# Transposing the new q and k in halves of 64 rows, q's upper rows beside k's lower rows

## What is computed

```python
q_rot, k_rot = (rotate(q), rotate(k))
scores = scale * np.matmul(q_rot, k_rot.transpose(0, 1, 3, 2))
scores = scores - np.max(scores, axis=-1, keepdims=True)
attn = np.exp(scores)
attn = attn / (np.sum(attn, axis=-1, keepdims=True) + 1e-09)
x = np.matmul(attn, v)                       # then heads side by side: 2304 x 512
h = x @ w_in                                 # 512 x 2048
g = np.maximum(h, 0.0) + alpha * np.minimum(h, 0.0)
out = g @ w_out
```

## Time and profile before

| | us |
|---|---|
| median of 2 runs | 701.41 (700.92 and 701.91) |
| the profiled execution | 700.88 |
| its span | 699.1 |
| TensorE products busy | 676.6 (97%) |
| VectorE busy | 372.4 (53%) |
| ScalarE busy | 314.2 (45%) |
| GpSimd busy | 282.1 (40%) |
| moved by the transfers | 51.30 MB |

### The profile page before, as it was taken

The page is one execution under the profiler, slowest core; times in us unless marked ns, Lnnn a source line. Parts: engine busy times, 40 slices in busy tenths (PEclk is TensorE's granted clock), DMA queues, the critical chain, the costliest instruction groups (busy, mean ns, idle before and its releaser), DMA issues.

```text
span 699.1 us, 12111 instructions
## 1 busy us (share of the span) xinstructions
PE 676.6 (97%) x4100; PEld 588.0 (84%) x4100; DVE 372.4 (53%) x681; ACT 314.2 (45%) x740; POOL 282.1 (40%) x258
## 2 busy tenths in 40 slices
PE   3899999999999999899999999999999999999996
PEld 3788888888888887698889999999999999999995
DVE  4688888888888878445642333233233323432231
ACT  2777777777777776333332222322322232223222
POOL 6655777777776504122222222222222222222221
PEclk9999999999999999999999999999999999999999
DMA  6897656666666642600001000000000010001001
GB/s 154 220 225 195 147 135 140 142 146 143 143 143 145 148 106 79 239 1 0 1 1 46 0 1 16 31 0 1 30 15 0 0 43 2 0 0 46 2 0 46
DMA packets 76619, 51.30 MB, mean 73 GB/s; under 512 B 61088, under 2 KB 61472, under 8 KB 76064
## 3 DMA queue, kind: packets, MB, share of 16 engines
q1 hardware_dynamic: 76576, 50.76, 28.9%
HBM read 22.95 MB, written 4.72 MB: 40 GB/s over the span
## 4 chain that ended last, share of the span: by engine, by line
PE 76%; issue 16%; POOL 2%; DVE 2%; DMA 1%; ACT 1%; SPq 1%; POOLq 0%; DVEq 0%; ACTq 0%
PE banks L620 19%; PE banks L647 19%; PE banks L547 14%; PE banks L505 12%; PE banks L566 10%; POOL g_lo L449 2%; PE banks L562 2%; DVE nmax L846 1%; DMA k_two<-k_hi 0%; DMA cos_sb<-in_cos 0%; DMA out<-stage 0%; DVE pt L895 0%; DVE k_lo L871 0%; ACT stage L807 0%; SPq L294 0%
## 5 line engine op out<-in xcount | busy, mean ns | idle before, releaser
L449 POOL TENSOR_TENSOR g_lo<-g,g_hi 128x384 fp32r<-128x384 f32 x96 | 99.3, 1035 | 312.2 <-ACT g_hi L795 306.1
L960 DVE TENSOR_SCALAR g<-banks,alpha_sb 128x384 f32<-128x384 f32 x96 | 59.3, 618 | 249.1 <-ACT pos L787 249.1
L620 PE MATMUL banks<-x_hi,w_in_lo 128*128 128x384 f32 x384 | 129.3, 337 | 0.0
L620 PE MATMUL banks<-x_hi,w_in_hi 128*128 128x384 f32 x384 | 129.2, 336 | 0.0
L620 PE MATMUL banks<-x_lo,w_in_hi 128*128 128x384 f32 x384 | 129.0, 336 | 0.0
L787 ACT ACTIVATE pos<-banks 128x384 f32<-128x384 f32 x96 | 47.1, 491 | 169.1 <-PE banks L620 169.1
L846 DVE TENSOR_REDUCE nmax<-banks 128x1 f32<-128x576 f32 x144 | 108.6, 755 | 22.8 <-PE banks L505 17.6
L647 PE MATMUL banks<-w_out_hi,g_hi 128*128 128x512 f32 x288 | 114.9, 399 | 1.6 <-POOL g_lo L449 1.4
L647 PE MATMUL banks<-w_out_hi,g_lo 128*128 128x512 f32 x288 | 112.9, 392 | 0.0
L647 PE MATMUL banks<-w_out_lo,g_hi 128*128 128x512 f32 x288 | 111.9, 389 | 0.0
L795 ACT ACTIVATE g_hi<-g 128x384 fp32r<-128x384 f32 x96 | 50.5, 526 | 119.7 <-DVE g L963 119.7
(11 more groups left out here) (83 smaller groups left out, 909.8 us busy)
## 6 DMA issues: line engine op xcount, KB each, us to landing
k_two<-k_hi SPq DMA_DIRECT2D x64, 160.0 KB, 2.9
out<-stage SPq DMA_DIRECT2D x18, 256.0 KB, 2.0
raw_q<-in_q SPq DMA_DIRECT2D x32, 128.0 KB, 2.8
raw_k<-in_k SPq DMA_DIRECT2D x32, 128.0 KB, 2.4
q_two<-q_hi SPq DMA_DIRECT2D x32, 128.0 KB, 2.3
q_two<-q_lo SPq DMA_DIRECT2D x32, 128.0 KB, 2.3
q_own<-q_hi SPq DMA_DIRECT2D x32, 128.0 KB, 2.4
raw_v<-in_v SPq DMA_DIRECT2D x32, 128.0 KB, 2.3
```

The lines of the kernel that those rows point to most:

```text
L449: nc.gpsimd.tensor_tensor(g_lo[f % 2][:, :], g[f % 2][:, :], g_hi[f % 2][:, :].bitcast(F32), ALU.subtract).then_inc(g_lo_done, 1)
L620: mm = nc.tensor.matmul(h_ps[f % 2], w[:, j, cols], xx[:, j, :], start=(step == 0), stop=(step == 3 * CT - 1))
L960: nc.vector.tensor_scalar(g[f % 2][:, :], h_ps[f % 2], 0.0, alpha_sb[:, f:f + 1], ALU.min, ALU.mult).then_inc(neg_done, 1)
```

## The change

The eight transposes of U_Q and U_K (four blocks each, 128 rows by 128 columns) become sixteen of 64 rows by 128 columns. The moving operand is then a 64x64 corner of the identity, and one instruction fills 64 of the block's columns in the bank. They are made by a new function, `turn_new`, in two steps of eight: step 0 takes rows 0 to 63 of q and rows 64 to 127 of k in turns, step 1 takes the other two halves. Q's halves go to U_Q's bank (1) and k's to U_K's bank (2), so that neighbouring instructions use different rows of the array and different banks.

In a period, step 0 stands between A1 and U_PB[3], and step 1 between U_PB[3] and A2; U_MIXED stands directly behind A2, where U_K's transposes were before it. Ahead of A1 come the waits of both units: that both banks are free and that both `rot_q` and `rot_k` are ready. Between the two steps, ahead of U_PB[3], TensorE waits on a new semaphore, half_turned, that the last product of step 0 raises. The semaphore `turned` is raised by 2 at the end of step 1. At the start, for pair 0, the two steps follow each other, and both rotations are waited for first.

```diff
--- before.py
+++ after.py
@@ -217,7 +217,7 @@
         scored = sem("scored")
         max_done = sem("max_done")
         exp_done = sem("exp_done")
-        turned = sem("turned")
+        turned, half_turned = sem("turned"), sem("half_turned")
         hi_done = sem("hi_done")
         evac = [sem(f"evac{i}") for i in range(T_BANKS)]
         sum_done = sem("sum_done")
@@ -528,12 +528,6 @@
                 elif u == U_INV:
                     pe.wait_ge(wide_done, p)
                     blocks = [inv_wide[:, i, :] for i in range(QT)]
-                elif u == U_Q:
-                    turned_in(p, 0)
-                    blocks = [rot_q[:, i, :] for i in range(QT)]
-                elif u == U_K:
-                    turned_in(p, 1)
-                    blocks = [rot_k[:, i, :] for i in range(QT)]
                 else:
                     blocks = []
                     if has_next(p):
@@ -546,6 +540,24 @@
                     i = 2 if at else i
                     mm = nc.tensor.transpose(bank[:, i * P:(i + 1) * P], block_in, ident[:, :])
                 mm.then_inc(turned, 1)
+
+            def turn_new(p, t, step):
+
+                if not exists_now(p, U_Q):
+                    return
+                bank_q, bank_k = t_ps[U_Q % T_BANKS], t_ps[U_K % T_BANKS]
+                if isinstance(p, int) and p == -1:
+                    if step:
+                        pe.wait_ge(half_turned, 1)
+                    else:
+                        turned_in(p, 0)
+                        turned_in(p, 1)
+                low, high = slice(0, D), slice(D, P)
+                for i in range(QT):
+                    for bank, rot, rows in ((bank_q, rot_q, high if step else low), (bank_k, rot_k, low if step else high)):
+                        mm = nc.tensor.transpose(bank[:, i * P + rows.start:i * P + rows.stop], rot[rows, i, :],
+                                                 ident[rows, rows])
+                mm.then_inc(turned if step else half_turned, 2 if step else 1)
 
             def pv(p, par, h):
 
@@ -581,11 +593,18 @@
                 turn(p, t, U_PB[0])
                 turn(p, t, U_PB[1])
                 turn(p, t, U_PB[2])
+                if exists_now(p, U_Q):
+                    fill(p, U_Q)
+                    fill(p, U_K)
+                    turned_in(p, 0)
+                    turned_in(p, 1)
                 score(p, t, A_TILES[1])
+                turn_new(p, t, 0)
+                if exists_now(p, U_Q):
+                    pe.wait_ge(half_turned, p + 2)
                 turn(p, t, U_PB[3])
-                turn(p, t, U_Q)
+                turn_new(p, t, 1)
                 score(p, t, A_TILES[2])
-                turn(p, t, U_K)
                 turn(p, t, U_MIXED)
                 score(p, t, A_TILES[3])
                 if not has_now(p):
@@ -661,8 +680,9 @@
                     output(i, c, FT - 1)
 
             pe.wait_ge(ident_in, 16)
-            for u in (*OF_NEXT, U_MIXED):
-                turn(-1, -1, u)
+            turn_new(-1, -1, 0)
+            turn_new(-1, -1, 1)
+            turn(-1, -1, U_MIXED)
             pe.wait_ge(padded, PADDED)
 
             def batch(b):
```

## The result

The changed kernel takes 740.8 us as the median of two runs (739.56 and 742.04) against 701.41: a ratio of 1.0565 (95% interval 1.0531 to 1.0598). Timed again among the experiments it took 740.32 us over five runs, 733.19 to 743.36, a ratio of 1.0575 (1.0547 to 1.0603). That spread of 10 us, where the kernel before has 2, is part of the result: it comes from TensorE's clock.

The account below looks back on a forecast made before the run. TensorE, busy 97% of the span, was taken to bound the kernel. Fourteen periods at 2.02 us (28.3) plus 4.5 for the start, 32.8 on the profiled 700.88, gave 734 us; range 726 to 746.

Parts of the forecast that it names:

- the clock: Rival: idle 1.5 us each period drops TensorE's clock to 1.2 GHz, 1.5 us more per period, 755 us; chance 0.03.
- a period over 19 us: Sign that would make the prediction wrong; it expected a period of 18.6 us instead of 16.62.
- The bound: Middle periods: only TensorE's pieces on the chain of waits, so anything added to its queue lengthens the kernel one for one.
- The moved wait: A1's first product waits for ScalarE's copy of U_PB[2] out of bank 2; TensorE stands still 1.51 us a period.
- the 0.03 for the release: Time from the end of ScalarE's copy of U_PB[2] to A1's new start: 0.03 us.
- Changes of division and halves: Per period: four changes, half_turned wait included, 0.78 us; sixteen halves 0.60 (0.44 to 0.87); eight whole transposes saved, 0.87.
- the fear of the issue of 32 short instructions: Halves put at 0.6 us, not 0.44: 32 short loads and products must issue in the time of fewer than eight before.
- A middle period: Each of periods 1 to 14 grows by 2.02 us (1.72 to 2.29); fourteen give 28.3 us.
- The start: Start and period 0: A1 waits for rotated k, and shifts behind it add up to 4.5 us, ends 3 and 7.
- 1 us net: At the start, behind A1: halves with their changes and wait add some 1 us at TensorE's lower clock.
- the 0.9 of slack in the transfers: At the start, SyncE reached q's copies late, so 0.9 us of TensorE's delay would be taken up.
- the rival that followed from it: Halves cost as much as whole transposes because weight loads set the pace: 16 us more, 750 us; chance 0.09.

Follow-up runs that it names:

- e12: The changed kernel itself timed again, no edit: 740.32 us over five runs, 733.19 to 743.36; its execution without a clock fall spans 731.4 us.
- e1: The kernel before with only the waits for banks 1 and 2 and both rotations moved ahead of A1, transposes whole and in place: 726.72 us.
- e9: Against e3: halves in one stretch behind A2, lower rows to bank 1, upper to bank 2, no wait between; start as in the kernel before: 704.71 us.
- e3: The changed kernel with both steps behind A2, a whole transpose between them, and the bank and rotation waits on A2's last product: 713.68 us.
- e5: The changed kernel with the wait for half_turned carried by the last of U_PB[3]'s four transposes instead of the first: 733.83 us.
- e6: e3 with rows 0 to 63 of both q and k in step 0 and rows 64 to 127 of both in step 1: 723.15 us.
- e11: e3 with whole transposes in the old places at the start and in period 0, halves from period 1 on: 710.74 us.
- e10: The changed kernel with A1's four products made two extra times ahead of the moved waits, filling the idle stretch: 735.15 us.
- e7: e1 with three tiny activations ahead of ScalarE's copy of U_PB[2], lengthening TensorE's idle stretch: 734.62 us, runs from 730.64 to 739.38.
- e4: The changed kernel with four halves of q queued ahead of four of k in each step, instead of in turns: 742.40 us.
- e2: The changed kernel with its moved waits carried by the last of A1's four products instead of the first: 729.95 us.

## Why the prediction held, and where it didn't

The forecast was 734 us with a range of 726 to 746; the result is 740.8. That it lies inside is in part luck: the bounds added up from the terms ended at 740, the widening to 746 was for dearer halves, and what brought the result there is the clock, which had 3 in 100. One of the prediction's own signs of being wrong came true: a period over 19 us, in six periods of the profiled execution.

*The bound.* TensorE was alone on the chain, and what was added to its queue came out one for one. From period 14's U_INV to the end the kernel before takes 442.4 us (256.75 to 699.1) and e12 442.4 (289.02 to 731.4), so nothing was added behind the last period that the change touches.

*The moved wait,* 1.51 us forecast: e1 measures 1.79 in a middle and 1.55 in an end period, as what it adds to the period. The mechanism and ScalarE's run of five are as described (the copy ends 3.01 us after the run's start, in both traces). The mis-sized term is the 0.03 for the release: in the loop A1 starts 0.31 us after the end of the copy. In the unlooped code it is 0.11, by e12's timeline and chain: the copy is done at 244.18 + 0.61 = 244.79, and A1's piece begins at 244.90:

```profile
244.18 0.61 ACT L764 ACTIVATE pt<-banks 128x512 f32<-128x512 f32 x1
```

```profile
244.90 0.77 PE banks L505 x4
```

I had taken what a wait on a single thing shows; A1 now waits on four semaphores, in the loop against values in registers. That this is what takes the time is likely and not tested.

*Changes of division and halves,* 0.78 + 0.60 - 0.87 = 0.51 forecast: 18.82 - 18.41 = 0.41 against e1, and 18.58 - 18.17 = 0.41 in end periods. No run prices one change alone, but the terms fit: e9 and e3 differ by two changes and the wait, 0.44, where the forecast had 0.30 + 0.16. The halves took 8 x 0.06 = 0.48, nearer to the bound of 0.44 than to my 0.6; the fear of the issue of 32 short instructions was wrong. The wait for half_turned is smaller than its share (e5: 0.1 of the 0.30).

*A middle period,* 2.02 forecast: 2.16 as the mean of 13 in e12 ((289.02 - 44.92 - 256.75 + 40.69) / 13).

*The start,* 4.5 forecast: 2.7 at the first stacked tile of period 1 (2.5 in e12, at 34.80). A1 of period 0 came at 20.44 where 20.5 was said. The mis-sized term is the "1 us net" for the halves and their changes behind A1: they cost nothing up to A2 and save 0.8 up to A3, because k's first halves run beside A1's products and k's whole transposes are gone. No run shows that the 0.9 of slack in the transfers was used: A3 is 2.76 late and the first tile of period 1 2.67. The clock's part in it I can't separate.

*The sum,* 32.8 forecast, 32.3 in the execution without a fall: 2.5 for the start and 29.8 for the fourteen periods, where 4.5 and 28.3 were forecast. The start too long by 2 us and the periods too short by 1.5 nearly cancel, which is luck.

*The clock.* This is the step that failed. I gave a falling clock 3 in 100, on the ground that "the stall is short, and TensorE works on all sides of it". The price in that rival, 1.5 us a fall, was right (1.55); it happens, but in six of 14 periods in one execution and in none in another, and the 7 us by which the median is above the forecast are its doing. What the runs show of the cause: without an idle stretch no period fell (e3, e6, e9, e11, clocks of 0.999 and 1.00); with it filled by repeated products none fell (e10); with 1.53 us of it and whole transposes none in four runs (e1), with 0.27 us more some (e7); with 1.53 us and the halves behind it some (changed kernel, e4, e12), and with 1.04 us and the halves still one (e2). So in these kernels a fall in the middle periods needs the idle stretch. That at 1.5 us the halves tip it is what e1 against the changed kernel suggests; by which property of theirs isn't shown. Why one period falls and its like in another execution doesn't stays open.

*The rules of the Trainium skill.* "TensorEngine Tiling (Array Packing)" in the Trainium skill says in "Key Properties" that a change of the tiling mode drains the engine; the traces agree in so far as the changes cost time, with the 0.16 us each that the trace of before already had fitting the sum. "TensorE: Matmul & The Clock Gate" in the Trainium skill says in "LDWEIGHTS" that a load's time goes by its columns, not its rows: the trace agrees, a half's load lasts 139 ns where a whole one's lasts 141. But it didn't set the pace, and the rival that followed from it fell.

## What to carry to other kernels

A wait that is moved ahead of other work holds all that work: before moving one, look up when the thing waited for is done, here a copy that was done 0.4 us before its old place (151.88, where U_K's loads began at 152.31) and 1.5 us late for its new one. Cutting a product to half the array pays only if the saving (0.4 us here) covers entering and leaving that division (0.16 each way), so such products belong in one stretch with no wait inside. And count a recurring idle stretch of 1.0 to 1.8 us on TensorE, as in these kernels, as more than its length: its clock may fall behind it, in some executions and not in others.

## What the runs showed of the hardware

Products on the lower and on the upper 64 rows of the array run as two streams that don't keep to the order of the queue, so that "in program order", as said of all engines at the beginning, doesn't hold for them: in e4 four halves of q were queued ahead of four of k, and the first of k started 10 ns after the first of q, while eight halves on the same rows took 0.24 us longer (e6). A score tile's products do the same: in period 0 the first half of k started at 21.30, ahead of A1's last two products at 21.54 and 21.78, behind which it was queued. "TensorE: Matmul & The Clock Gate" in the Trainium skill says, in "The mechanism", that products start and end in the order of the program; these rows of starts don't agree. So the order in the queue can't be relied on to keep two such streams apart; the changed kernel uses a semaphore, e9 a bank for each.

The clock fell to half for some 3.4 us, some 2 us after work had resumed behind an idle stretch of only 1.5 us (1.04 in e2), and came back while the work went on. The time it adds, 1.55 us a fall, differs between executions by up to 10 us in all, which a pair of runs can't tell from the effect of an edit; the granted clock of each run tells it.
